# A hand-written order with four mixing slots per period gets three, one of them moved behind the last group

## The reference

```
# layer 1, for each batch and head, over the 768 tokens in order
y[t]  = r[t] @ state
Sa    = state @ a[t]
state = state * w[t] - outer(Sa, b[t]) + outer(v[t], k[t])
# layer 2: mixing along the tokens (rank 32), then along the channels (320 -> 1280 -> 320)
u = x + (x.T @ U @ V).T
x = u + relu(u @ w_ch1) @ w_ch2
# layer 3: causal attention with 4 experts of width 64, the top 2 of a gate weigh them
out = sum_e gate_e * softmax(mask(q_e @ k_e.T / 8)) @ v_e @ wo_e
```

## Time and profile before

| of the profiled execution | |
|---|---|
| time of this execution | 1120.31 us |
| span from first to last instruction | 1118.5 us |
| PE (matmul) busy | 1030.7 us, 92% |
| PEld (weight load) busy | 755.2 us, 68% |
| DVE (VectorE) busy | 585.9 us, 52% |
| ACT (ScalarE) busy | 431.9 us, 39% |
| POOL (GpSimd) busy | 324.2 us, 29% |
| mean granted TensorE clock | 0.977 of 2.4 GHz |

### The profile page before, as it was taken

One profiled execution on the slowest core, in us unless ns is written; L12 is line 12 of the kernel. 1 busy time (PEld: TensorE's weight loads), 2 busy tenths in 40 slices (PEclk: granted clock), 3 DMA queues, 4 the chain that ended last, 5 costly groups with the idle time before them and its releaser, 6 DMA issues. The chain is left out here.

```text
span 1118.5 us, 51461 instructions
## 1 busy us (share of the span) xinstructions
PE 1030.7 (92%) x23136; PEld 755.2 (68%) x23136; DVE 585.9 (52%) x1288; ACT 431.9 (39%) x1207; POOL 324.2 (29%) x564
## 2 busy tenths in 40 slices
PE   4888877999999898899999899899999898999987
PEld 3777766667666787666766787666766687655556
DVE  6887773434335886343334787433334776210275
ACT  3766652222122565422222555422212455310155
POOL 4554554223223443122332434212222330000000
PEclk9998997999999999999999999899999999999989
DMA  8232333124212231111211222101210111000000
GB/s 232 77 107 87 102 94 96 36 69 120 77 42 65 71 95 50 61 41 49 65 60 47 80 72 81 58 25 50 59 45 24 50 55 42 21 1 1 1 13 25
DMA packets 47993, 68.37 MB, mean 61 GB/s; under 512 B 19744, under 2 KB 34848, under 8 KB 47776
## 3 DMA queue, kind: packets, MB, share of 16 engines
q1 hardware_dynamic: 47776, 65.09, 19.8%
HBM read 57.19 MB, written 7.86 MB: 58 GB/s over the span
## 5 line engine op out<-in xcount | busy, mean ns | idle before, releaser
L568 POOL TENSOR_TENSOR QI<-R,consts 128x256 f32<-128x256 f32 x180 | 135.6, 764 | 342.9 <-DVE R L787 321.5
L787 DVE COPY R<-PB 128x512 f32<-128x512 f32 (+1 forms) x147 | 95.5, 654 | 72.6 <-PE PB L1060 62.3
L663 ACT COPY R<-PB 128x512 f32<-128x512 f32 (+1 forms) x111 | 64.8, 584 | 153.6 <-PE PB L1060 146.7
L1347 PE MATMUL PB<-uf,W 128*128 128x384 f32 x320 | 112.4, 497 | 0.7 <-issue 0.7
L1379 PE MATMUL PB<-work,W 128*128 128x384 f32 x320 | 109.5, 493 | 0.0
L1052 PE MATMUL PB<-R 64*64 64x64 f32 x4032 | 85.1, 225 | 10.5 <-DVE UP L846 4.3
L1052 PEld LDWEIGHTS PB<-R 64*64 64x64 f32 x4032 | 71.0, 137 | 33.7 <-issue 21.8
L1347 PEld LDWEIGHTS PB<-uf,W 128*128 128x128 f32 x320 | 58.0, 189 | 46.3 <-issue 12.2
L975 DVE TENSOR_SCALAR work<-PB 128x384 f32<-128x384 f32 x40 | 22.3, 557 | 118.3 <-PE PB L1354 61.6
L1379 PEld LDWEIGHTS PB<-work,W 128*128 128x128 f32 x320 | 58.9, 190 | 37.5
L754 ACT COPY work<-PB 128x512 f32<-128x512 f32 (+3 forms) x128 | 53.2, 444 | 55.7 <-PE PB L1444 55.1
(11 more groups left out here) (154 smaller groups left out, 2133.8 us busy)
## 6 DMA issues: line engine op xcount, KB each, us to landing
EA<-ea_dram SPq DMA_DIRECT2D x48, 498.0 KB, 3.5
LA<-la_dram SPq DMA_DIRECT2D x48, 384.0 KB, 3.5
VT<-vt_dram SPq DMA_DIRECT2D x48, 80.0 KB, 2.9
x_mid_dram<-XO SPq DMA_DIRECT2D x192, 20.0 KB, 1.9
xs<-x_mid_dram SPq DMA_DIRECT2D x24, 160.0 KB, 3.5
out_dram<-work SPq DMA_DIRECT2D x24, 160.0 KB, 1.8
W<-w_dram SPq DMA_DIRECT2D x7, 320.0 KB, 4.7
W<-w_dram SPq DMA_DIRECT2D x1, 1280.0 KB, 10.1
```

The lines of the kernel that those rows point to most:

```text
L568: nc.gpsimd.tensor_tensor(QI[j][:].rearrange("p (u g t) -> p u g t", u=2, g=2), src.rearrange("p u (g t) -> p u g t", g=2), eye3.unsqueeze ...
L663: freed(nc.scalar.copy(tile[:, 8 * C:8 * C + hi], ps[:, 1, 0:hi]), group, i)
L787: freed(nc.vector.tensor_copy(tile[:, lo:hi], PB[PLACE[group, i][0]][:, 0, lo:hi]), group, i)
L1347: mm = nc.tensor.matmul(b_[:, j, 0:HW], W1[:, f, lo:lo + P], uf[:, f, j * HW:(j + 1) * HW], start=(f == 0 and m % 2 == 0), stop=(f == 1 an ...
```

## The change

The diff moves marks and adapts the three totals. No instruction, tile or semaphore is changed; the order in which the steps stand on all engines is.

```diff
-PERIOD = ("A1", "A2", "mix", "A3", "B1", "mix", "scan", "den", "B3", "B2", "mix", "C1", "C2", "mix", "C3", "inv", "bk")
+PERIOD = ("A1", "A2", "mix", "A3", "B1", "scan", "den", "B3", "B2", "mix", "C1", "C2", "C3", "inv", "bk", "mix")
...
-BESIDE_MIXING = (32, 27, 22)
+BESIDE_MIXING = (24, 20, 16)
```

## The result

The change made the kernel slower. Over nine runs each, the kernel before took 1115.28 us in the median (1113.39 to 1122.36; the three runs shown ahead of the prediction are among them) and the changed one 1124.78 us (1121.32 to 1129.34). The ratio is 1.0075 with an interval of [1.0049, 1.0100], which is 8.4 us of 1115.28 (the medians themselves lie 9.5 apart). The executions profiled took 1120.31 us before and 1127.87 us after, spans of 1118.5 and 1126.1 us, both from the upper half of their kernel's runs.

What follows compares the result with a forecast made beforehand. It took PE, busy nearly throughout the mixing stretches, as the bound, so time there is the sum of its pitches. Terms 2.5 - 1.2 - 1.6 - 0.7 + 1.3 - 0.6 - 0.4 + 0.8 = +0.1 gave 1120.4 us, range 1116.3 to 1124.6.

Steps and rivals of the forecast that it cites:

- no effect that can be seen: Whole kernel: the summed terms give 1120.4 us, with a range of its own from 1118.3 to 1122.4; chance 0.48.
- Feeding PE, +0.8: Run A3, B1, B3, B2: two packet borders in some 8 of 19 runs, 0.1 us each, +0.8 us; bounds 0 and 4.8.
- Rival A: End of B1 or B2 in mixing periods: feed stalls cost 4.8 us, not 0.8, giving 1124.4 us; chance 0.17.
- The join without the B mark, +2.5: Between B1 and B3 in mixing: joined groups, mostly B3's wait for WS, cost 18 x 0.14 = +2.5 us.
- even exit: Even step ending in 64-row products before B3 or C3: costs 0.15 us; eight such go, -1.2 us.
- The C mark: Mark between C2 and C3 moves behind C3: ways in and out stay two, 0.13 us to spare, costed at nothing.
- Rival B: C3 waits for C1's banks in each period: 20 x 0.14 = +2.8 us, giving 1123.2 us; chance 0.10.
- Empty marks, -1.6: Periods 17 and 20, A3 to next block: marks no longer empty, saving 0.81 + 1.23 less 0.2 each, -1.6 us.
- h 0 of batch 0, -0.7: Step behind the last u: C1, C2, C3 now stand between and cover its 0.70 us wait for DVE's sum, -0.7 us.
- First scores, +1.3: First score in batches 0 and 1: now directly behind the last qk, it waits 0.65 us each, +1.3 us.
- The attention stretches, -0.4: Batch 2 gains A3 and B1 (0 to -1.8), batch 0 loses C3 as cover (0 to +0.6); a third of each, -0.4 us.
- Rival C: Batch 2 attention absorbs A3 and B1 wholly (-1.8) and first scores' +1.3 goes, giving 1117.7 us; chance 0.23.

Runs made afterwards that it cites:

- The run with 21 marks: Kernel before with 21 marks instead of 22 for batch 2, ending its mixing one mark earlier, against the kernel before: 1111.93 us, 0.9971 [0.9947, 0.9996].

## What held in the prediction and what failed, by its own steps

It gave 1120.4 us, "no effect that can be seen", and the kernel got 0.75% slower. Its sum was +0.1 us, and the kernel took 8.4 us more. The median of 1124.78 us lies 0.2 us above its range (up to 1124.6), and that it is so near is luck: the base it started from, 1120.31 us, was itself 5 us above the median of all nine runs of before. Two of the signs that it gave for being wrong came true in the profile: mixing stretches longer by over 3 us (3.1 and 3.3), and an attention stretch that moved by over 2 (5.2).

**Feeding PE, +0.8: the step that failed.** The prediction found the right mechanism, packets of 256 instructions, and took its effect from the number of borders in one run of groups. Two things were wrong. The place: it looked at A3, B1, B3, B2 alone. There the changed kernel lost 0.39 + 1.26 us in two periods and had no such wait in the others, twice the 0.8 put down for it. (Rival A had over 0.4 us in each of some eight; it named the right place for these two, and not for the 2.03 us.) The other two stalls (0.86 and 2.03 us) stand behind C1, C2, C3, 148 matmul records with as many loads. That run was there before the change too, with 144 records, so it is not the move of the C mark that made it fast: a border now falls at its end. And the base: the prediction costed the borders that the new order would meet, but not that the kernel before met its own at a favourable place. This is the part of 4.5 us, and the runs with 64 to 256 more instructions show it. No reading of the one trace gives it, but that the change moves every border behind 185 us could be seen, and it should have widened the range; 0.17 for "the feed stalls" was too little.
The Trainium skill, in "Runtime: NRT & Kernel Launch", section "Instruction fetch mechanics", calls the cost of crossing such a border mostly hidden. The trace agrees with its 256 instructions of 16 KiB (184 packets of 3.01 MB, all stalls at one number modulo 256) and not with "hidden": 8.9 us of such waits in the profile of before, 14.2 in that of after.

**The clock had no term.** Behind the stall of 2.03 us PE ran at 0.50 for 3.20 us, and eight products took 4.54 us, not 2.85. A stall of the feed can so cost nearly double. It need not: of the seven stalls of over 1 us behind 205 us in this profile three (2.03, 1.57 and 1.56 us) have a granted clock of 0.50 within 2 us of their end, and four (1.18 to 1.53 us) have not. No run isolates this.

**The join without the B mark, +2.5: too small.** The mechanism held: in batch 1 B3 starts in each period 1.2 us behind B1, and 0.06 behind WS in period 28. The size did not. In period 28 B1 to what follows it takes 1.23 us against 1.04, and B3 to B2 0.80 against 0.75: 0.24 where I had 0.14. The period took 0.29 more in all, and no even step stands in front of B3 or C3 in it, before or after. I had split the same 0.29 us of period 15 into 0.15 for an even exit and 0.14 for the join, and that split does not hold here. For seven periods of batch 1 it is 2.0 us and not 1.0. Some 0.05 us of the 0.29 are left for the next point.

**A missing term: ways into odd steps.** I wrote that even and odd steps cost the same at the new places. They do not: a step that begins with 64-row products directly behind C3's transposes starts 513.70 - 513.12 = 0.58 us behind them, a step that begins with 128-row products 0.49, and `h` 7 itself takes 517.33 - 513.70 = 3.63 us to the next A1. Batch 1 has four such places (490.58, 513.70, 582.32 and 605.91), each 0.58 us behind C3: with 0.09 each they are some 0.4 us, in part counted in the 0.29 above.

**A missing term: x2_first waits for DVE.** With three marks in a period in place of four the blocks are larger, and in batch 1 the first step of x2 comes directly behind `h` 9, whose banks DVE's L975 has still to empty: 0.75 us at 531.52. All five profiles of the order after have it, and the trace without the B mark (0.8 us each); the one with the C mark moved has not, and before has no idle time there. It could be had from the planned weights: I went through them for marks that stay empty, not for steps that come together in one block. (That the larger blocks are the cause is argued from the order of the steps; no run takes it apart.)

Together mixing 1 is 2.5 to 5.3 us longer in the order after (149.5 to 152.0 us at the five places, against 146.7 to 147.0). It is the one stretch that is longer at every place. By my terms it should have been 1.0 + 0.65 = 1.65 longer; with 2.0 for the join, 0.75 for x2_first and no wait at the score, 2.75 of the 3.3 us in the first two profiles are accounted for.

**The C mark.** C3 did not wait for C1's banks: 513.12 - 511.99 = 1.13 us behind C2, no idle time. Rival B is out.

**Empty marks, -1.6.** Right in place, open in size: periods 17 and 20 have no idle time at A3 and B1 any more. The waits that stood there were two borders, though, and no run shows what an empty mark costs by itself. Mixing 0 is 1.2 us shorter wherever no border falls badly, and with C3 of period 21 taken in. My terms for this stretch make about -0.3 (-1.6, -0.75 for five even exits, +0.8 for six joins, +0.65 for the score, +0.6 for C3), so they miss some 0.9 us of gain.

**h 0 of batch 0, -0.7.** The wait for DVE's sum went, as predicted, and an "issue" wait of 0.86 us stood in its place. A gain from cover is only a gain if what fills it does not bring PE to the next border too early.

**First scores, +1.3.** Half of it. Batch 0 waits 0.65 us (361.58), batch 2 as before (877.71), but batch 1 does not wait at all: its score stands directly behind qk at 622.91. A1 of period 22 lost its 0.59, as predicted (362.00).

**The attention stretches, -0.4: too small in batch 2.** Attention 2 took in A3 and B1 (1.79 us) and was not longer for it: 87.3 to 89.7 us at the five places, against 88.4 to 93.5 in the order before. Mixing 2 gave the time up: 135.1 to 136.3 us against 136.8 to 137.8. The run with 21 marks shows this part alone, 0.29% or 3.2 us faster [0.4 to 5.9]. Rival C was right in this mechanism; the interval holds its 1.8 us and more. It hid part of the price of the rest. In attention 1, where no order changed, the profile after has 5.2 us more; in the others both orders have 95.8 to 101.0. Its waits after (first three) and before (last two):

```profile
PE PB L1087 <- issue: 2.3, 2, 1.6
...
PE PB L1052 <- issue: 1.9, 2, 1.5
...
PE PB L1040 <- issue: 1.2, 1, 1.2
```

```profile
PE PB L1052 <- issue: 2.2, 2, 1.3
...
PE PB L1087 <- issue: 0.5, 1, 0.5
```

These are borders that fall otherwise, not an effect of the order there.

**What stays open.** Whether there is a part that does not hang on the place, and how its 3.8 us divide among the stretches; how much goes by way of the clock; and why some packets start late behind a slow block. Mixing 1 is 3.5 us longer in the mean of the five profiles of each order, but mixing 2 (-1.3) and attentions 0 and 2 (-2.0 and -2.5) are shorter, and all stretches from mixing 0 to attention 2 together have 756.9 us after against 757.8 before. The times say that the order after is slower, these sums don't. There is one profile of each kernel, most runs of one kernel lie within 0.5% of its median either way, and a profiled one need not be typical: with 128 more the order after took 1120.15 us in its profile and 1129.63 in the median. And with four places the 0.34 +- 0.19% tell little of a fifth place; at 64 the new order was not slower.

## What to carry to other kernels

Where small instructions follow each other at full pace, an "issue" wait is often the end of an instruction block. Count the engine's instructions modulo 256, and look when the queue's last packet started, before looking for any other cause. A reordering moves all borders behind it: before a difference of under 1% is put down to an order, both orders should be timed at several places of the borders, with a shift by a whole packet as the control. And an edit late in the program, as the 21 marks here, can be judged more cleanly than an early one, since everything ahead of it stays where it was.

## What the hardware showed that I had not expected

- Adding 64 PE instructions, some 0.1% of them, at 12 us into the program made it 0.74% slower; adding 256 made it 0.14% slower, within its interval of no change.
- All 232 "issue" waits of PE of 0.1 us or more between 205 and 1000 us in 14 profiles stand at instruction 193 to 195 modulo 256, and no border whose packet had started over 2.83 us ahead of PE has one. They last up to 2.85 us, the longest in mixing 0 with 256 more instructions:

```profile
357.51 1.31 PE L1410 MATMUL PB<-ur,WQ 64*128 64x384 f32 x4 [2.85 <-issue]
```

- A stall of 2.03 us was followed by 3.20 us at a granted clock of 0.50.
